# A branch on SyncE placed in front of the last wait for outputs, and the flag read earlier on every busy engine

## The reference

```python
for t in range(S):                                   # linear attention with decay
    cur = einsum('bhd,bhe->bhde', u * k[t], v[t])
    y[:, :, t] = einsum('bhd,bhde->bhe', r[t], state + cur)
    state = w * state + einsum('bhd,bhe->bhde', k[t], v[t])
...
expert_idx = argmax(x @ w_gate)                      # 8 experts, one per token, capacity 384
h = maximum(disp @ w1, 0); y = h @ w2                # 384 -> 1024 -> 384 per expert
out[i] = gate_w[i] * y[expert_idx[i], pos[i]]        # tokens over capacity stay zero
...
h = x @ w_in                                         # 384 -> 2048
g = h * clip(h + 3, 0, 6) / 6
return g @ w_out                                     # 2048 -> 384
```

## Time and profile before

| | |
|---|---|
| median of 3 timed runs | 463.49 us (463.0, 463.49, 466.93) |
| the profiled execution | 460.62 us, of which the span 458.9 |
| PE busy | 427.3 us, 93% of the span |
| mean granted clock of PE | 0.97 |
| chain that ended last | PE 72%, issue 9%, POOL 7%, DVE 5% |

### The profile page before, as it was taken

The page is one execution under the profiler, slowest core; times in us unless marked ns, Lnnn a source line. Parts: engine busy times, 40 slices in busy tenths (PEclk is TensorE's granted clock), DMA queues, the critical chain, the costliest instruction groups (busy, mean ns, idle before and its releaser), DMA issues.

```text
span 458.9 us, 7418 instructions
## 1 busy us (share of the span) xinstructions
PE 427.3 (93%) x2810; PEld 365.3 (80%) x2810; DVE 248.8 (54%) x500; ACT 211.5 (46%) x481; POOL 76.6 (17%) x85
## 2 busy tenths in 40 slices
PE   6798987879899999999998999999999999999992
PEld 4577876667899999999886788887788887888872
DVE  5687885464889679678647333333423333332331
ACT  1455547544668568567557323334322344332230
POOL 3876875120110210210200000000000000000000
PEclk8898889799999999999999999999999999999998
DMA  7999993248375865965954100001000001000002
GB/s 186 246 301 315 323 320 107 69 147 297 134 268 196 325 218 179 343 200 185 305 173 159 60 0 1 0 1 69 1 0 0 1 0 69 1 1 1 0 0 74
DMA packets 28699, 60.56 MB, mean 132 GB/s; under 512 B 2334, under 2 KB 19401, under 8 KB 28659
## 3 DMA queue, kind: packets, MB, share of 16 engines
q1 hardware_dynamic: 26866, 55.30, 37.6%
q0 software_dynamic: 1792, 4.73, 2.7%
HBM read 49.77 MB, written 11.04 MB: 133 GB/s over the span
## 4 chain that ended last, share of the span: by engine, by line
PE 72%; issue 9%; POOL 7%; DVE 5%; DMA 2%; ACT 2%; SPq 1%; POOLq 0%
PE ps L1514 22%; PE ps L1516 22%; PE ps L1515 21%; PE ps L1541 3%; POOL rk L639 2%; POOL rku L645 2%; POOL kt_sc L632 2%; DMA x_stage<-y_dram 1%; PE ps L1667 1%; PE ps L1577 1%; DVE w_lo L1148 1%; DMA xg<-xs_dram 1%; DVE w_lo L1092 1%; SPq L410 1%; DVE rk_sc L992 1%
## 5 line engine op out<-in xcount | busy, mean ns | idle before, releaser
L1241 DVE SCALAR_TENSOR_TENSOR u_sb<-t_sb,ps 128x512 f32<-128x512 f32 x48 | 33.0, 689 | 121.9 <-ACT t_sb L899 121.8
L899 ACT ACTIVATE t_sb<-ps,three 128x512 f32<-128x512 f32 x48 | 33.0, 689 | 117.3 <-PE ps L1516 117.2
L1514 PE MATMUL ps<-h_hi,w_hi 128*128 128x512 f32 x144 | 57.5, 399 | 0.9 <-DVE h_lo L1247 0.8
L1516 PE MATMUL ps<-h_hi,w_lo 128*128 128x512 f32 x144 | 56.8, 395 | 0.0
L1514 PE MATMUL ps<-x_hi,win_hi 128*128 128x512 f32 x144 | 56.7, 394 | 0.0
L1515 PE MATMUL ps<-x_lo,win_hi 128*128 128x512 f32 x144 | 56.3, 391 | 0.0
L1516 PE MATMUL ps<-x_hi,win_lo 128*128 128x512 f32 x144 | 56.2, 390 | 0.0
L1515 PE MATMUL ps<-h_lo,w_hi 128*128 128x512 f32 x144 | 56.0, 389 | 0.0
L1514 PE MATMUL ps<-w_hi,h_hi 128*128 128x384 f32 x128 | 43.7, 341 | 1.8 <-DVE h_lo L1121 1.8
L1516 PE MATMUL ps<-w_hi,h_lo 128*128 128x384 f32 x128 | 42.9, 335 | 0.0
L1515 PE MATMUL ps<-w_lo,h_hi 128*128 128x384 f32 x128 | 42.8, 334 | 0.0
(11 more groups left out here) (141 smaller groups left out, 806.9 us busy)
## 6 DMA issues: line engine op xcount, KB each, us to landing
raw<-in_w SPq DMA_DIRECT2D x16, 1536.0 KB
tm_in<-in_krv_tm SPq DMA_DIRECT2D x12, 576.0 KB, 11.3
dm_in<-in_rk_dm SPq DMA_DIRECT2D x12, 448.0 KB, 14.5
xs_dram<-fill SPq DMA_DIRECT2D x2, 1544.0 KB, 10.7
raw_in<-in_w_in SPq DMA_DIRECT2D x8, 384.0 KB
raw<-in_w_out SPq DMA_DIRECT2D x2, 1536.0 KB, 9.5
xg<-xs_dram SPq DMA_DIRECT2D x7, 386.0 KB, 7.1
x_stage<-y_dram SPq DMA_DIRECT2D x3, 768.0 KB, 4.6
```

The lines of the kernel that those rows point to most:

```text
L899: nc.scalar.activation(t_sb[n % 2][:, :], ps[:, 3 + n % 3, :], ACT.Relu, bias=three[:, 0:1]).then_inc(t_done, 1)
L1241: nc.vector.scalar_tensor_tensor(out=u_sb[n % 2][:, :], in0=t_sb[n % 2][:, :], scalar=6.0, in1=ps[:, 3 + n % 3, :], op0=ALU.min, op1=ALU.m ...
L1514: mm(o, a_hi, b_hi, start=first, stop=False)
L1516: return mm(o, a_lo, b_hi, start=False, stop=last)
```

## The change

The flag is read into the register earlier on four engines. On SP, the wait for `s_verdict` and the load stand in front of the stores (behind the loads of `x_stage`). On ACT and DVE they stand in front of the three `mlp_block`s, behind the splits of `w_out`; on PE in front of the transposes of the first block of `x_stage`. POOL is unchanged. The branches of ACT, DVE and PE stay behind the last `mlp_block`. On SP the branch stands behind the last store, and the wait for the stores' landing behind the branch, in a block of its own; on the general path the same wait also stands at its head.

```diff
--- before.py
+++ after.py
@@ -510,17 +510,17 @@
                 sp.wait_ge(y_sent[0], 16 * E)
                 sp.wait_ge(y_sent[1], 16 * (E - 1 if q == 0 else E))
                 sp.dma_start(x_stage[:, q * BLK:(q + 1) * BLK, 0:D], y_rows[q]).then_inc(ld_y[q], 16)
+            sp.wait_ge(s_verdict, 1)
+            good = sp.value_load(flags[0:1, 0:1], min_val=0, max_val=1)
             for q in range(NB):
                 for i in range(DC):
                     sp.wait_ge(o_moved[i], q + 1)
                     sp.dma_start(out[q, i], o_sb[i][:, :]).then_inc(o_stored[i], 16)
-            for i in range(DC):
-                sp.wait_ge(o_stored[i], 16 * NB)
-
-
-            sp.wait_ge(s_verdict, 1)
-            good = sp.value_load(flags[0:1, 0:1], min_val=0, max_val=1)
+
+
             with sp.If(good < 1):
+                for i in range(DC):
+                    sp.wait_ge(o_stored[i], 16 * NB)
                 sp.dma_start(w_bc[:, :], w_row[0, :].partition_broadcast(DH)).then_inc(slow_wu, 16)
                 sp.dma_start(u_bc2[:, :], u_row[0, :].partition_broadcast(DH)).then_inc(slow_wu, 16)
                 sp.dma_start(all_wg[:, :, :], w_gate.rearrange("(c p) e -> p c e", p=P)).then_inc(all_wg_in, 16)
@@ -929,12 +932,12 @@
                 x2_split_hi(0, k)
             for k in range(FC, F2C):
                 wo_split_hi(k)
+            act.wait_ge(s_verdict, 1)
+            good = act.value_load(flags[0:1, 0:1], min_val=0, max_val=1)
             for q in range(NB):
                 mlp_block(q, q == NB - 1)
 
 
-            act.wait_ge(s_verdict, 1)
-            good = act.value_load(flags[0:1, 0:1], min_val=0, max_val=1)
             with act.If(good < 1):
                 for j in range(NT):
                     act.wait_ge(all_route, 5 * j + 2)
@@ -1271,12 +1274,12 @@
                 x2_split_lo(0, k)
             for f in range(FC, F2C):
                 wo_split_lo(f)
+            dve.wait_ge(s_verdict, 1)
+            good = dve.value_load(flags[0:1, 0:1], min_val=0, max_val=1)
             for q in range(NB):
                 mlp_block(q, q == NB - 1)
 
 
-            dve.wait_ge(s_verdict, 1)
-            good = dve.value_load(flags[0:1, 0:1], min_val=0, max_val=1)
             with dve.If(good < 1):
 
                 dve.wait_ge(slow_wu, 32)
@@ -1707,14 +1710,14 @@
                 project(q, F2C * q + F2C - 2, F2C - 2)
                 project(q, F2C * q + F2C - 1, F2C - 1)
 
+            pe.wait_ge(s_verdict, 1)
+            good = pe.value_load(flags[0:1, 0:1], min_val=0, max_val=1)
             for k in range(DC):
                 turn_x2(0, k)
             for q in range(NB):
                 mlp_block(q, q == NB - 1)
 
 
-            pe.wait_ge(s_verdict, 1)
-            good = pe.value_load(flags[0:1, 0:1], min_val=0, max_val=1)
             with pe.If(good < 1):
                 pe.wait_ge(slow_x, 16)
                 pe.wait_ge(all_wg_in, 16)
```

## The result

With the change, 12 timed runs have a median of 457.35 us (454.80 to 463.77); 12 runs of the kernel before, 461.62 (457.87 to 466.93). The ratio is 0.994, 95% interval 0.9914 to 0.9965: 2.8 us less, between 1.6 and 4.0. The ratio and its interval are taken from the fast runs alone, the medians from all.

The account below looks back on a forecast made before the run. PE was taken as the bound, busy 427.3 of 458.9 us, so only its idle time or the end matter. SyncE's 3.4 us less and DVE's 0.6 more sum to -2.8: 463.49 to 460.7 us, range 459.4 to 463.7.

Parts of the forecast that it names:

- 0.5 from the runs: Part of the forecast's range: the spread of the timed runs before, 463.0 to 463.49 us.
- the 2 to 3.4 that I had named: Sign for the whole program: the prediction is wrong if the span doesn't shrink by 2 to 3.4 us.
- SyncE's branch, 3.4 us less: At the end: with flag load and branch ahead of the last wait, SyncE's drain moves from 458.6 to 455.2.
- the cover: At the end: SyncE's branch stall finishes before the last store lands at 455.2, with 0.2 to 0.8 us to spare.
- the second jump: At SyncE's end: the jump after the last wait costs nothing; rival, another 2.5 us, 463.2, chance 0.12 shared with another stall.
- DVE's load, 0.6 us more: Start of the last stage: DVE's flag load between w_lo and u_sb delays the chain to PE by 0.6 us.
- DVE has no cover: Start of the last stage: DVE's flag load stands in the chain PE waits for, priced at 0.6 us.
- My lower bound of 0.3: DVE's load by ACT's row: issued behind the last w_lo at 251.7, 0.8 us to the branch, delay 0.3 us.
- PE's and ACT's loads: Start of the last stage: both cost zero; PE at worst 0.1 us, ACT 0.3 without DVE's own delay.
- The stall is something else's: Rival at SyncE's end: the drain's 2.5 us are not the branch's; 463.2 us, chance 0.12 shared with the second jump.
- Clock: Rival after PE's longer gap at 253.6: granted clock halves, costing 3.5 us, 464.2 us; chance 0.04.
- DVE hidden: Rival at the last stage's start: DVE's load hides, with ACT's overlap; 460.4 us and below, chance 0.04 with more gained.

Follow-up runs that it names:

- e4: The kernel before with SyncE's general path cut to its first three transfers; one profiled execution, 6.50 us from the last matmul's start to the last semaphore.
- e3: The kernel before without flag load, branch and general path on all five engines; ratio 0.9877 to before.
- e10: The change with SyncE's branch ahead of all stores, DVE's and PE's ahead of the last block; ratio 0.9859 to before, 6 runs.
- e11: e10 with PE's last 18 matmuls ordered by output part in addition; ratio 0.9881 to before.
- e15: e10 with PE's branch moved to behind its first three tiles; ratio 0.9937 to before.
- e18: e10 with PE's branch moved inside the last block, behind the tenth tile's first product; median 456.49 us, ratio 0.9879 to before, 6 runs.
- e12: The change with PE's general path cut to one wait; one profiled execution, 4.92 us from the last matmul's start to the last semaphore.
- e14: The change with PE's last 18 matmuls ordered by output part; ratio 0.9832 to before, from 7 runs.
- e6: The change with a wait for the last w_lo's end before DVE's flag load; profiled only, 11.05 us from first transposes to second product's first matmul.
- e5: The change with DVE reading the flag four times instead of once; profiled only, 11.74 us from first transposes to second product's first matmul.
- e2: The change with SyncE's wait for the stores again ahead of its branch; ratio 0.9977 to before.
- e17: The change with SyncE's and DVE's branches moved early, PE's left behind the last block; ratio 0.9941 to before.
- e1: The change on SyncE alone, PE, ACT and DVE reading the flag at their end as before; ratio 0.993 to before.
- e13: The change with DVE's general path cut to one wait; one profiled execution, 5.33 us from the last matmul's start to the last semaphore.

## Why the prediction was wrong

**The time was wrong because of its level.** The step that failed is the last one of the sum, 463.49 - 2.8 with "0.5 from the runs" for its range: 463.49 is a median of three runs. Single runs on one chip spread over 11 us, five medians of 12 to 35 runs of the same kernel lie between 461.35 and 463.51, and the three runs were 1.9 above the 12. Of the 3.3 us by which the median is below my 460.7, 1.9 are the level of before. The difference of the two medians is 4.3 instead of 2.8, while the ratio gives 2.8 and the last stage in the traces 3.1: the rest of the miss is the spread of medians, but for 0.3. The row that would have warned me was there: the profiled execution stood 2.9 below the median, and I noted it and did not widen the range for it. The range does not follow from its own terms either: 460.7 with 0.3 less on DVE and 0.5 from the runs is 459.9, not 459.7 or 459.4, and upward 0.7, 0.4 and 0.5 more make 462.3, not 461.7. Added up rightly it would have missed too.

**Where the numbers came out, luck had a part.** The same terms taken off the profiled execution gave 457.8, and it took 457.99. But in that execution the last stage is 3.1 us shorter, not 2.8, and it began 0.5 us later than before (244.83 against 244.36), which no term has. The 2.8 of the ratio agrees with the 2.8 of the sum, and with 1.6 to 4.0 it can't tell -3.4 + 0.6 from -3.2 + 0. The span shrank by 2.6, inside the 2 to 3.4 that I had named.

**SyncE's branch, 3.4 us less: right in its mechanism, measured 3.2 (2.7 to 3.2 over four executions of the change, against the one of before).** The 2.5 us are the branch's (e4), the cover is the landing (wait until 455.8, branch at 452.5), and the second jump is free (38 ns and 0.1 us behind it), as the start of the program had shown. The Trainium skill's rule in "Runtime: NRT & Kernel Launch", section "Instruction fetch mechanics", that a taken branch to code outside the pages held waits for its fetch, agrees with the 2.5 us over the whole general path and the 0.2 over its first three transfers (e4).

**What I took for granted there is wrong: that the store's landing is a fixed 3.6 us.** In the kernel before 1.6 of it come with the code that PE and DVE load at the same time (the wait is 3.3 us there, 3.1 to 3.9 in all executions with the branches at the end, and 1.7 in e3, e10, e11, e15 and e18). The cover of SyncE's branch is thus made in part by code loading itself: in e12 and e14, where the stores land earlier, the branch is the end. I had read the packets of kind "instruction" as a sign of the stall alone, not as traffic in the way of the stores.

**DVE's load, 0.6 us more: wrong, measured 0.0.** The step that failed is "DVE has no cover". I took the end's row, where the load had nothing queued ahead of it but one instruction. In the middle the sequencer had two `w_lo` handed over and unfinished when it reached the load. My lower bound of 0.3 let the load start with the last `w_lo`; it started 0.6 us ahead of that. The price without that lead is 1.0 (e6). PE's and ACT's loads: zero, as said; they ran at 241.0 and 248.0, well ahead.

**The rivals.** Second jump: no. The stall is something else's: no (e4). Clock: not with the change, but it came in e5, with a longer gap. DVE hidden: yes, this was the case, given 0.04 with others; its price was off too, since hidden whole it leaves 463.49 - 3.4 = 460.1, not 460.4.

## What to carry over

A median of three is no level when single runs spread by over 1%: forecast the difference, and give the range of a time the spread of medians. A register load costs nothing where the sequencer is ahead of its engine by the load's 0.8 us, and 1 us directly behind a wait. A branch over long code costs its stall and also traffic: put it where the sequencer is some 4 us ahead (PE's stall was up to 3.8 at the end, 5.5 beside heavy loads) and no store is being waited for.

## What the runs showed of the hardware

- A taken branch over the whole general path stalls SyncE 2.5 us in quiet (before, e2) and 2.9 to 3.1 beside the stores (e14, e12), DVE 2.8 to 3.5, PE 3.3 to 3.8. Beside the loads of `x_stage` it is 5.5 on PE at 256 GB/s (e15) and 5.2 to 5.9 on SyncE (e10, e11, e15, e17, e18). Over a few instructions it takes 0.2 on SyncE (e4).
- With packets of code (8 and 16 KB) among them the 768 KB of the last stores land later: their last packet ends 2.8 us after the last matmul's start without any, 3.6 without PE's, 4.3 to 5.0 with PE's (in e14, where two of the three stores go out earlier, 3.6); SyncE's wait is 1.7 us without any and 3.1 to 3.9 with PE's.
- A register load in a row behind another takes 0.30 us (e5), alone 0.46 to 0.55, and 0.80 to 0.82 on DVE when it begins beside the last `o_sb` (before, e1, e4).
- PE's granted clock fell to half for 3.4 us in e5 after PE had stood still for 2.47 us, and in e3, e13 and e18 at 247.2, behind waits of 0.6 us for `x_stage` and 1.07 for `x_lo`; in the other executions with these two waits it stayed at full, and so it did behind waits of 1.5 to 1.8 us in e6, e10, e11 and e15.
